# Expert shares multiplied at the way out of PSUM, y summed in DRAM by adding transfers, ReLU on ScalarE, operand sums on VectorE

## What is computed

```python
scores = scale * np.matmul(q, k.transpose(0, 1, 3, 2))      # batch 4, heads 8, seq 576, head_dim 64
attn = softmax of the scores where block_i >= block_j (blocks of 64)
x = np.matmul(attn, v), laid out as (2304, 512)

p = domain_probs / (domain_probs.sum(-1, keepdims=True) + 1e-09)
for e in range(4):                                          # w1[e]: 512 x 1024, w2[e]: 1024 x 512
    h = np.maximum(x @ w1[e], 0.0)
    out += p[:, e:e + 1] * (h @ w2[e])

h = out @ w_in;  solu = h * softmax(h);  layer norm with g_ln;  result = ln @ w_out
```

## Time and profile before

| | us |
|---|---|
| median of three executions | 1228.89 |
| the profiled execution | 1228.42 |
| its span, first to last instruction | 1226.4 |
| TensorE busy in the span | 1126.9 |
| VectorE busy | 919.7 |
| GpSimd busy | 646.4 |
| ScalarE busy | 507.3 |
| phases 0 to 11, from the first down product of phase 0 | 215.8 to 1016.8 |

### The profile page before, as it was taken

How to read it: one execution, slowest core, us unless ns; L and a number is a source line. 1 busy time by engine, 2 the same in 40 slices (tenths; PEclk the granted TensorE clock), 3 DMA queues, 4 the chain that set the end, 5 groups by cost and what they waited for, 6 DMA issues and landing times.

```text
span 1226.4 us, 17666 instructions
## 1 busy us (share of the span) xinstructions
PE 1126.9 (92%) x6331; PEld 1062.8 (87%) x6331; DVE 919.7 (75%) x1078; ACT 507.3 (41%) x922; POOL 646.4 (53%) x412
## 2 busy tenths in 40 slices
PE   8999999589987989998997989798998979999998
PEld 7999998489886979988897989797998977888887
DVE  8999976966749785767868494968567698676775
ACT  8998983232333332233333224223222343343332
POOL 8998985944748571136664052746204655234220
PEclk9999999789998989999898999999999999999999
DMA  5767778259291645626373625355461622111100
GB/s 160 222 220 232 245 264 293 78 206 333 78 345 59 198 141 170 196 81 216 111 241 108 203 93 177 110 179 169 144 221 53 196 95 78 43 35 61 43 26 35
DMA packets 102328, 188.85 MB, mean 154 GB/s; under 512 B 8723, under 2 KB 52827, under 8 KB 102253
## 3 DMA queue, kind: packets, MB, share of 16 engines
q1 hardware_dynamic: 101820, 187.81, 46.4%
q10 hardware_dynamic: 432, 0.07, 0.0%
HBM read 138.19 MB, written 49.66 MB: 153 GB/s over the span
## 4 chain that ended last, share of the span: by engine, by line
PE 43%; DVE 15%; issue 11%; ACT 2%; DMA 1%; SPq 0%; DVEq 0%; ACTq 0%
PE s L2276 20%; PE ring L2276 10%; PE outp L2137 8%; DVE spare L1859 7%; PE outp L2276 4%; DVE t L1846 2%; DVE acc L1884 2%; ACT spare L1478 1%; DVE h L1836 1%; PE ring L2410 1%; DMA ring_x<-x_stash 1%; DVE h L1823 1%; DVE h L1830 1%; DVE h L1817 1%; DVE acc L1882 0%
## 5 line engine op out<-in xcount | busy, mean ns | idle before, releaser
L2276 PE MATMUL ring<-spare,w2s 128*128 128x384 f32 x1152 | 217.1, 342 | 30.7 <-DVE spare L1859 27.1
L1478 ACT ACTIVATE spare<-h 128x768 fp32r<-128x768 f32 x144 | 121.0, 844 | 282.3 <-DVE h L1823 98.9
L2276 PEld LDWEIGHTS ring<-spare,w2s 128*128 128x128 f32 x1152 | 203.7, 191 | 37.9 <-DVE spare L1859 26.4
L1859 DVE TENSOR_TENSOR spare<-h,spare 128x768 fp32r<-128x768 f32 x144 | 179.8, 1266 | 26.6 <-ACT spare L1478 25.3
L2276 PE MATMUL s<-ring_x,w1s 128*128 128x384 f32 x1056 | 194.3, 339 | 3.4 <-DMA ring_x<-x_stash 3.4
L2276 PEld LDWEIGHTS s<-ring_x,w1s 128*128 128x128 f32 x1056 | 186.7, 188 | 4.4 <-DMA ring_x<-x_stash 4.3
L1160 POOL TENSOR_TENSOR h<-h,t 128x768 f32<-128x768 f32 x22 | 51.1, 2324 | 193.5 <-DVE t L1846 193.5
L1154 POOL TENSOR_TENSOR w1s<-raw_w,w1s 128x1024 fp32r<-128x1024 f32 x28 | 76.5, 2745 | 81.2 <-ACT w1s L1462 81.2
L1830 DVE SCALAR_TENSOR_TENSOR h<-h,share 128x768 f32<-128x768 f32 x72 | 114.4, 1627 | 0.0
L2276 PE MATMUL s<-spare,w2s 128*128 128x384 f32 x576 | 107.6, 339 | 6.2 <-DVE spare L1859 5.7
L2276 PEld LDWEIGHTS s<-spare,w2s 128*128 128x128 f32 x576 | 100.6, 190 | 11.6 <-issue 7.1
(11 more groups left out here) (184 smaller groups left out, 2424.1 us busy)
## 6 DMA issues: line engine op xcount, KB each, us to landing
ring_x<-x_stash SPq DMA_DIRECT2D x154, 384.0 KB, 3.8
y_rows<-acc SPq DMA_DIRECT2D x48, 384.0 KB, 2.6
raw_w<-in_moe_w SPq DMA_DIRECT2D x28, 512.0 KB, 7.4
acc<-y_rows SPq DMA_DIRECT2D x36, 384.0 KB, 5.8
r_sb<-r_scratch SPq DMA_DIRECT2D x16, 576.0 KB, 4.2
x_rows<-x_n SPq DMA_DIRECT2D x32, 288.0 KB, 4.5
x_rows<-x_rows SPq DMA_DIRECT2D x16, 384.0 KB, 4.9
x_stash<-grain SPq DMA_DIRECT2D x15, 384.0 KB, 4.9
```

Source lines behind the costliest of these rows:

```text
L1478: act.activation(spare[number % SPARE][:, 0:PAIR_COLS], t2[:, :] if source is None else half_of(source, h), ACT.Copy).then_inc(op_high, 1)
L1859: dve.tensor_tensor(part[:, PAIR_COLS:2 * PAIR_COLS], t2[:, :] if source is None else half_of(source, h), part[:, 0:PAIR_COLS].bitcast(f32 ...
L2276: last = pe.matmul(target, x, y, start=start and i == 0, stop=stop and i == 2, skip_group_check=True)
```

## The change

Four things are changed together.

1. **Shares.** h is no longer multiplied by the share. `fold` and `last_block` are gone. `flush` multiplies the product by the share where it leaves PSUM, and writes it to one of three stage buffers of 384 KB. m5 and m3 are multiplied by -1 as well, since t1 and one of the differences of w2 (S4) now have the other sign.
2. **y.** The four `acc` quarters, `store_acc` and `load_acc` are gone. GpSimd issues a transfer for each of the seven flushed products (`send`), which adds it to its quarter of y in DRAM. The first one of each quarter in phases 0 to 2 is plain, 12 of the 84. A send waits for the flush, and for the send before it into the same quarter to have landed. A flush waits until the send of the flush three places back has landed, since it reuses its buffer.
3. **ReLU.** h12 and h21 are rectified on ScalarE (`rectify_h12`, in place in SBUF; `rectify_h21`, out of PSUM). For h11 and h22 the ReLU is inside the instructions that read them: `operand_high` with ACT.Relu, and a scalar_tensor_tensor with op0 = max on VectorE.
4. **Sums.** `make_t3` and `make_t4` go from GpSimd to VectorE. GpSimd keeps the weight differences and low parts.

```diff
@@ SyncE
-            def load_acc(n):
...
-            def store_acc(n, i):
...
             def load_share(n):
...
-                    sp.wait_ge(op_low, operand_no(n - 1, "m6", 1))
-                    sp.wait_ge(t4_made, halves(n - 1, 1))
+                    sp.wait_ge(flush_done, flushed(n - 1, "m4"))
@@ GpSimd
+            def send(n, name):
+                mine, later = kept(n, name)
+                pool.wait_ge(flush_done, flushed(n, name))
+                if later > 16:
+                    pool.wait_ge(mine, later - 16)
+                target, source = y_dram[n % SUPERS, FLUSH[name]], stage[stage_at[n, name]][:, :]
+                if n < SUPERS and name in FIRST_FLUSH:
+                    pool.dma_start(target, source).then_inc(mine, 16)
+                else:
+                    pool.dma_start(target, source, accum_op=ALU.add).then_inc(mine, 16)
...
+            for n in range(SUPERS, PHASES):
+                e, sg = n // SUPERS, n % SUPERS
+                send(n - 1, "m4")
+                if sg == 0:
+                    prepare(job2(e), (A11, A12, S2, S1, S3, S4, A22))
+                if sg == SUPERS - 1:
+                    prepare(job1(e + 1), (A11, A12, S2, S1, S3))
+                send(n, "m1")
+                if sg == SUPERS - 1:
+                    prepare(job1(e + 1), (S4,))
...
+                send(n, "m2")
+                if sg == SUPERS - 1:
+                    prepare(job1(e + 1), (A22,))
+                for name in ("m6", "m5", "m7", "m3"):
+                    send(n, name)
@@ ScalarE
+            def rectify_h12(n, h):
+                act.wait_ge(up_added, added(n, "m3", h))
+                act.activation(half_of(h12, h), half_of(h12, h), ACT.Relu).then_inc(rectified, 1)
+            def rectify_h21(n, h):
+                act.wait_ge(up_done, upped(n, "m4", 2 * h + 1))
...
+                act.activation(half_rows(h21, h), two_banks(banks_up("m4", h)), ACT.Relu).then_inc(rectified, 1)
@@ VectorE
             def make_t1(n, h):
-                dve.wait_ge(folded, folded_no(n, "h12", h))
+                dve.wait_ge(rectified, rectified_no(n, "h12", h))
                 dve.wait_ge(op_low, operand_no(n, "m1", h))
...
             def flush(n, name):
...
+                if user is not None:
+                    dve.wait_ge(*kept(user[0], user[1]))
...
+                    dve.tensor_tensor(target, source, share_of(quarter % 2), ALU.mult).then_inc(flush_done, 1)
             def first_layer(n):
...
-                for h in range(2):
-                    fold(n, "h11", "m2", h)
...
                 for h in range(2):
+                    make_t1(n, h)
+                make_t2(n, 0)
             def second_layer(n):
+                operand_low(n, 2)
+                make_t4(n, 0)
+                operand_low(n, 3)
+                flush(n, "m1")
+                operand_low(n, 4)
```

More of the change, by code:

```diff
@@ L181, in build_program @@
         ring_x = [put(f"ring_x{s}", [P, PAIR_COLS], f32r) for s in range(RING)]
-        acc = put("acc", [P, 8 * GROUP])
+        at_t2 = place["at"]
+        t2 = put("t2", [P, PAIR_COLS])
+        stage = [put(f"stage{s}", [P, PAIR_COLS]) for s in range(3)]
         at_h = place["at"]
@@ L190, in build_program @@
         at_free = place["at"]
-        place["at"] = at_share
-        t2 = put("t2", [P, PAIR_COLS])
+        assert at_free == at_h - PAIR_COLS * 4
         place["at"] = at_raw_w
@@ L267, in build_program @@
         sums1_late = put("t_late1", [P, 3 * GROUP])
-        place["at"] = at_free - PAIR_COLS * 4
-        grain_acc = put("grain_acc", [P, PAIR_COLS], f32r)
         place["at"] = at_raw_w
@@ L1221, in y_add, with prepare @@
+            def prepare(job, ks):
+                for k_ in ks:
+                    if k_ in (A11, A12):
+                        w_difference(job, 0 if k_ == A11 else 2)
+                    if k_ == A11:
+                        w_difference(job, 1)
+                    w_low_part(job, k_)
+                    if k_ == S3:
+                        w_difference(job, 3)
             def y_add(p):
@@ L1240, in y_add @@
                 pool.tensor_tensor(t4, b21, t2, ALU.subtract).then_inc(y_summed, 1)
+            late_sum(0)
+            late_lows(0)
+            w_difference(0, 2)
+            w_low_part(0, A12)
+            late_sum(1)
+            w_difference(0, 3)
+            send(0, "m1")
+            late_lows(1, range(2))
+            send(0, "m2")
+            late_lows(1, (2,))
+            send(0, "m6")
+            late_lows(1, (3, 4))
+            send(0, "m5")
+            late_lows(1, (5,))
+            send(0, "m7")
+            late_lows(1, (6,))
+            send(0, "m3")
+            late_sum(2)
+            send(0, "m4")
+            late_lows(2)
+            send(1, "m1")
+            late_sum(3)
+            send(1, "m2")
+            send(1, "m6")
+            late_lows(3, range(2))
+            send(1, "m5")
+            late_lows(3, (2,))
+            send(1, "m7")
+            late_lows(3, (3, 4))
+            send(1, "m3")
+            send(1, "m4")
+            late_lows(3, (5, 6))
+            prepare(job1(1), (A11, A12, S2))
+            send(2, "m1")
+            prepare(job1(1), (S1,))
+            send(2, "m2")
+            prepare(job1(1), (S3,))
+            send(2, "m6")
+            prepare(job1(1), (S4,))
+            send(2, "m5")
+            prepare(job1(1), (A22,))
+            send(2, "m7")
+            send(2, "m3")
+            for n in range(SUPERS, PHASES):
[8 more added lines that the diff above has]
+                    prepare(job1(e + 1), (S4,))
+                if n == PHASES - 1:
+                    y_add(0)
+                send(n, "m2")
[3 more added lines that the diff above has]
+                    send(n, name)
             def y_low_rows(p):
@@ L1491, in first_layer @@
                     cast_late(0, range(4, NP))
+                    for h in range(2):
+                        rectify_h12(n, h)
                     return
@@ new lines, in flush @@
+                target = stage[stage_at[n, name]][:, :].rearrange("p (c x) -> p c x", c=2)
+                source = two_banks(banks_down(name))
+                if name in NEGATIVE:
+                    dve.scalar_tensor_tensor(out=target, in0=source, scalar=-1.0, in1=share_of(quarter % 2),
+                                             op0=ALU.mult, op1=ALU.mult).then_inc(flush_done, 1)
+                else:
+                    dve.tensor_tensor(target, source, share_of(quarter % 2), ALU.mult).then_inc(flush_done, 1)
@@ L1963, in second_layer @@
                 flush(n, "m7")
+                if last:
+                    y_low_sums(0)
                 operand_low(n, 12)
```

304 lines of the change are left out of this document (102 added, 202 removed).

## The result

The changed kernel takes **1172.28 us** (median of 4 runs, 1170.49 to 1173.67) against 1229.08 for the kernel before on the same chip: a ratio of 0.9536, 95% interval 0.9519 to 0.9552. That is faster, inside the predicted range of 1128 to 1195, outside the forecast's 1137 to 1165 that had a chance of 0.50, and 25 us above the predicted 1147. The profiled execution has a span of 1169.9 us in place of 1226.4, so 56.5 us went and not 81. A second measurement on another chip gave 1170.40 and a ratio of 0.9512 (0.9499 to 0.9525).

A forecast was written before the change was run, and what follows sets the result against it. TensorE has most work but is held from outside, at the up-to-down turn and inside m6. Savings 24 + 21 + 15 + 7.5 + 5 + 8 = 81 us off 1228.4 give 1147 us; range 1128 to 1195.

The forecast's parts named there:

- The bound and the place: TensorE, busy 92%, is held from outside, at the turn from up to down and inside m6; unheld phase 58.8 us.
- Its signs of being wrong: Flushes wait for DMAs, m6 waits 3 us for low parts everywhere, or ScalarE's ReLU holds the turn.
- w2 phases, 21: Phases 3, 6, 9: stall ahead of m2 falls from 5.97 to 1.8 us; 61.7 for 68.7, 21 us saved.
- No job, 15: Phases 4, 7, 10: the 2.11 us stall inside m6 and smaller ones go; 63.8 to 58.9, 15 us saved.
- w1 phases, 24: Phases 5, 8, 11: no stall ahead of m2, 1.5 us of waits inside m6; 24 us saved.
- Phase 0, 8: Phase 0, 54 us: VectorE loses folds and last blocks ahead of m2; 8 us saved, between 0 and 15.
- Phases 1 and 2, 12.5: Phase 1 falls from 66 to 61, 5 saved; phase 2 saves 7.5 of 77 as x grains come earlier.
- Second layer, 0: Nothing counted for attention and the second layer: instructions unchanged, except y loaded in 4 pieces for 2.
- L: Time from flush to landing of an adding transfer: taken as 6 us, costing nothing up to 8.6.
- The slower rival: Adding transfers land too late, holding m7's flush; 18 us per us past 8.6, phases 3 to 11; chance 0.13.
- GpSimd issues late beside VectorE: A send waits for a gap in VectorE's work, 3 us on top of L; 7 us, 1154; chance 0.05.
- New waits eat half: Each phase keeps a 3 to 4 us stall from VectorE's ring with ScalarE's ReLU and t3, t4; 1185; chance 0.20.

The follow-up runs named there:

- E6: Changed kernel with ScalarE's two ReLUs of h12 ahead of the last two casts in the w2 phases (3, 6, 9); 1166.28 us, ratio 0.9490.
- E4: Kernel before with only t3 and t4 of phases 1 to 11 moved to VectorE; 1210.04 us, ratio 0.9826.
- E5: Changed kernel with GpSimd's last low parts of a w1 job (phases 2, 5, 8) behind the send of m6 or later; 1174.07 us, ratio 0.9552.
- E9: Changed kernel with the last low parts of the weight jobs (S4, A22) made on VectorE instead of GpSimd; 1156.91 us, ratio 0.9404.
- E1: Changed kernel with every transfer of a stage buffer a plain store instead of an adding one; 1163.50 us, ratio 0.9457.
- E7: Changed kernel with supergroup 2's row loads behind two ring loads, and the last grain's low part and row sum ahead of sends; 1169.56 us, ratio 0.9518.
- E11: Changed kernel with E8's and E9's edits, plus supergroup 2's row loads behind five ring loads and their sum behind phase 0's last send; 1167.21 us, ratio 0.9493.
- E8: Changed kernel with VectorE's end reordered: y low parts behind m3's last in phase 11, all w_out low parts before m4's flush; 1166.40 us, ratio 0.9477.
- E2: Changed kernel, every transfer made twice, first into a second y; theory A: free until 8.6 us, then 2 us a phase per us; measured 1224.10 us, ratio 0.9941.

## Why the prediction was right, and where its sizes were wrong

**The bound and the place.** Right. The loss sat at the turn and inside m6, and with the folds and sums gone the phases with no job fell to the unheld 58.8 us, the others to 60.9 and 61.6 to 61.9. Phases 3 to 11 were to give 60 us and gave 56. The 25 us that the prediction was short by lie mostly in the w1 phases (6.6), phases 1 and 2 (15.6) and the second layer (4.4); phases 3, 6 and 9 gave 2.7 more than written.

**Its signs of being wrong.** Of three, one came in full: the turn of phases 3, 6 and 9 is held by ScalarE's ReLU, and E6 shows what that costs, 0.9 us a phase. Flushes wait for DMAs in phase 0 alone, and m6 nowhere waits 3 us from phase 2 on. The lengths came out in another order, 60.9 for the w2 phases and 61.6 to 61.9 for phases 5 and 8, where 62 and 60 were written.

**w2 phases, 21.** Measured 23.7. The stall is 1.48 for 1.8, and it is the one described: t1 behind ScalarE's ReLU, which stands behind casts, and beside GpSimd. The 1.1 us for a slower clock behind it did not come: the granted clock is 1.00. E6 shows that 0.9 of the 2.1 us a phase that are left is the order on ScalarE.

**No job, 15.** Measured 14.9, and E4 shows that the sums on VectorE alone give 13.8.

**w1 phases, 24.** Measured 17.4. The turn came out as written, no stall ahead of m2. The term that was sized wrong is the 1.5 us for GpSimd's last two low parts: phases 5 and 8 lose 3.1 and 2.8, phase 11 loses 6.8. VectorE had just been given t3 and t4, each of which can be held for the whole of a GpSimd instruction. In phase 11 the low parts of y are held in the same way (2.17 us), ahead of the low part that m7 waits 3.29 us for. The prediction priced such a meeting at the turn, from the earlier trace rows, and took VectorE's 24 instructions of the down half at 0.87 each, though two in each w1 phase would meet GpSimd. E5 shows that one later place does not mend it, E9 that taking the work off GpSimd does in phases 5 and 8.

**Phase 0, 8.** Measured 8.0. The prediction took it between bounds of 0 and 15 without a sum, and no run splits it: that it fits is luck.

**Phases 1 and 2, 12.5.** Measured -3.1, the largest miss. In phase 1 TensorE waits for x from the ring:

```profile
271.57 2.29 PE L2277 MATMUL ring<-ring_x,w1s 128*128 128x384 f32 x6 [5.13 <-DMA ring_x<-x_stash]
```

The cause that suggests itself is a buffer. The change takes `acc` away, and with it the third grain buffer of supergroup 1's second half, and ScalarE waits for a stash transfer before it can make the last grain. But so it does in the kernel before, whose last four grains already took turns in two buffers. First the changed kernel, then the one before:

```profile
261.06 0.52 ACT L1449 ACTIVATE grain_tail<-t_late 128x384 fp32r<-128x384 f32 x1 [5.13 <-DMA x_stash<-grain_tail]
```

```profile
268.96 0.53 ACT L1443 ACTIVATE grain_ring<-t_late 128x384 fp32r<-128x384 f32 x1 [4.21 <-DMA x_stash<-grain_ring]
```

In both the last grain is made 0.9 us ahead of phase 1, which starts at 261.94 and at 269.89. What differs is how long the two ring loads behind it are under way. They are issued 1.2 and some 1.7 us into phase 1 in each kernel. The lines give the two loads' time from issue to landing, in the kernel before, in the changed one and in E1:

```profile
DMA to landing us min/median/max: 3.1/3.4/3.8
```

```profile
DMA to landing us min/median/max: 8.3/8.5/8.7
```

```profile
DMA to landing us min/median/max: 5.1/5.3/5.5
```

Beside them are two adding sends of phase 0, issued at 260.25 and 262.62, of which the second lands after 8.7 us. In E1, with plain sends, ScalarE's wait is 5.13 us as in the changed kernel and TensorE's is 1.82: the grain has not come sooner, the loads have landed sooner. So the step that failed is the transfers at no cost in phases 1 and 2. Their price was worked out against the stage buffers alone, and nothing was put down for the ring loads of phase 1, which are issued just when they are needed. E1 wins back 5 to 7 us in the two phases. What the missing buffer costs besides was not tried; ScalarE's wait is 0.9 us longer with it gone. The second loss of phase 1 is again a held sum, t2 of the second half beside GpSimd's sum of rows, which ends at 309.31:

```profile
305.68 4.46 DVE L1861 SCALAR_TENSOR_TENSOR t<-h,h 128x768 f32<-128x768 f32 x1
```

E4, which has the sums on VectorE and nothing else of the change, has longer waits for VectorE in this phase too. After these waits TensorE runs at the lower level for a while (granted clock 0.93 in phase 1, 1.00 before), which is 2.4 us more of busy time. In phase 2 a t3 is held for 5.96 us by two GpSimd instructions on the late weights; it ends at 390.66, 0.81 behind the second of them. E7 and E11 moved the row loads and mended nothing.

**Second layer, 0.** Measured -4.4, and -3.1 in the repeat. In the first profile four low parts of w_out take 5.82 us beside GpSimd, where they took 2.73, and `hu` behind them is late by 2.91. It was "instructions that do not change", but the meeting of two engines did. E8 gives 3.1 us of it back.

**The transfers.** L was taken at 6; from phase 3 on its median is 5.8, between 4.8 and 10.8, mostly 0.3 from the flush to the issue and 5.1 to the landing. Adding costs nothing in phases 3 to 10, as E1 shows (phase 11 is 0.3 us shorter in it). "No flush has a DMA as its releaser" holds from phase 1 on; in phase 0, with two stage buffers, the last two flushes wait 2.92 and 5.23 us for a landing, and TensorE feels neither. The Trainium skill (Collectives: The Full Stack, section on the bandwidth ceiling) says of the reducing step of a ReduceScatter that its add needs two source reads and so runs at half the rate. The time to landing here fits that, 5.1 us for the 2.7 of E1; what the engines read was not seen. The slower rival's price, 18 us for each us over 8.6, is near by luck. In E2 the sends of m1 land some 8 us and those of m2 some 12 us after their flushes, in place of 5.2 and 6.0, and phases 3 to 11 lose 40 us where E2's theory A says 43, but through the ring loads of the up half, which the prediction had only as a remark. The 22.5 behind the threshold of 8.6 was too early, since a flush of m7 at 24.2 cost m4 0.36 us.

**The rivals.** "GpSimd issues late beside VectorE" did not happen. The send of m1 in phase 5 starts 0.3 us after its flush ended, with VectorE at work on a low part. Where one starts later, GpSimd's own low part stands ahead of it (m2 in phase 5, 1.5 us) or the landing of an earlier send. The rule of the Trainium skill that stood beside it (SBUF — State Buffer, section on the two separate sides) speaks of a lock in VectorE's two-port modes, and no send here met one. "New waits eat half" was the nearest: the waits are real (t1 behind the ReLU, low parts behind t3), but in six of the nine phases from 3 on only, and 1.5 to 2.3 us each, 4.3 in phase 11. The measured 1172 lies between the forecast and this rival's 1185.

**The clock.** Predicted 0.98 for the phases. It is 1.00 in phases 3 to 5 and 0.93 to 0.97 in 1, 2 and 11, the phases with the longest waits (5.13, 4.05, 3.29 us): the product behind the wait of 3.29 in phase 11 takes 5.98 us for 4.3.

## What to carry to other kernels

When work is taken off the engine that is waited for, list next every pair of instructions that the new order puts side by side on VectorE and GpSimd; if both read two SBUF operands, the one that comes second waits for the end of the first, and of what follows the first without a gap (5.96 us behind two in phase 2). Moving the GpSimd instruction may only choose another sum to be held, as E5 did. Before you call new transfers free, look beyond the buffers that they fill, at the loads that are under way beside them in each phase: in phase 1 a load that took 3.1 us took 8.4. When a wait seems to have a cause, look for the same wait in the kernel before and in the other runs. And test a threshold where you say it is: a run that gives the predicted number may still get it at another place, as E2 did.

## What the runs showed of the hardware

- A 384 KB transfer that adds in DRAM lands 5.1 us after its issue at the median, a plain one 2.7 (E1), on the same queue. An adding send takes GpSimd 0.86 us, a plain one 0.57. With twice the adding traffic (E2) ring loads of the same size land after 8.0 us at the median for 3.1.
- A VectorE sum with two SBUF inputs ends 0.81 to 0.83 us behind the end of the GpSimd instruction beside it, in all five places told (phase 5 twice, phases 1 and 2, E5), and takes 2.48 to 5.96 us in all: held, not slowed. The flushes, with one input in PSUM and one in SBUF, take 0.94 to 0.96 us each, all 84 of them (the 48 of one kind have a mean of 953 ns).
- The 128x1024 low part of a weight block takes VectorE 1.22 us and GpSimd 2.41 at the median, up to 3.1. Beside VectorE's two-input sums the cheaper place for it is VectorE itself, as E9 shows in phases 5 and 8.
